# State products on four quarters of the array, logit sums one chunk later, column maxima joined on POOL

## The chip, the cores and the metric

The program runs on one core of a Trainium2 chip. The time is the device time of one execution in microseconds (us). Three runs of the kernel before took 564.08, 565.28 and 568.5 us; the median is 565.28 us.

## The reference

q, k and v have the shape 4 x 8 x 768 x 64 (batch, heads, sequence, head dimension), all float32. Three stages follow one another:

```
state = gamma[h] * state + k_t (outer) v_t ;  y_t = q_t . state / 8       # attention, per batch and head
x = y as 3072 tokens x 512
logits = x @ phi (512 x 32);  d = softmax over the 3072 tokens;  slot_input = d.T @ x
slot_out[e] = relu(slot_input[e] @ w1[e]) @ w2[e]                        # 8 experts, 4 slots each
x = softmax over the 32 slots of logits @ slot_out
out = sum over the top 2 of 8 experts (noisy gate) of weight * relu(x @ w1b[e]) @ w2b[e]
```

The first softmax runs over the tokens, so it needs a maximum for each of the 32 columns of the logits over all tokens.

## The kernel before, in words

**Chunks.** The sequence of each batch is cut into 6 chunks of 128 tokens, so there are 24 chunks, numbered t = 0 to 23. Chunk by chunk, attention is computed as products within the chunk and a product with the state that the earlier chunks left. The program is written out by hand for each engine; semaphores order the engines.

**TensorE, one chunk (`sequence_products`, L735).** In iteration t it issues, in this order: `scores` (L643) of chunk t+1, q.k for 8 heads with 64 contraction rows; `logit_parts_of` (L657) of chunk t-1, phi times x in four column tiles of 32; a wait for the state of this chunk (`state_ready`); `turn_x` (L675) of chunk t-1, four transposes of 128x128; `outputs`, which are the 8 state products (L684, not in the first chunk of a batch) and the 8 products of masked scores and v (L690), all into one bank of PSUM, `Y`; `logit_rows` (L664) of chunk t-1, which sums the four parts of the logits by one product with a stack of unit matrices; `update` (L697), the 8 products k.v for the state (not in the last chunk of a batch). Each float32 product shows as two records in the trace, so 8 products are x16.

**State products.** Head 2n uses the array's rows and columns 0 to 63, head 2n+1 rows and columns 64 to 127. Two of the four 64x64 quarters of the array are used.

**Other engines.** DVE masks the scores (L1182), scales y into `x_t` (`keep_x_t`, L1189) and keeps the state (`keep_state`, L1198 and L1201). ACT copies the logit parts (L1009), the turned x (L1015) and the logits (L1017). POOL scales v by its decay (L531). SP loads q, k and v, two transfers of 512 KB for a chunk (L408), and between them the first stage's w1 in halves of 1024 KB (L440), 14 halves for the 21 chunks from 3 on. A chunk's k and v are loaded when the scores of the chunk two before are done, its q and k-by-token when the update four before is done.

**Column maxima.** The chunks form five groups, which end before chunks 4, 8, 14, 20 and 24. For each group DVE finds the maximum over its chunks for each partition (`find_max`, L1222, and a copy to four places, L1224), TensorE turns it (`turn_max`, L704), DVE reduces it and joins it with the older maximum (`join_max`, L1230 to L1233), TensorE spreads it to all partitions (`spread_max`, L710), DVE subtracts (`shift_cols`, L1241), ACT takes the exponential (L1022, L1024), and TensorE sums the slots (L719) and denominators (L731). For the last group this chain has nothing of attention left beside it.

**After attention** the products with w1 (L808) and w2 (L830) of the slots follow, then the gate, the sort by expert and the second expert stage (L940, L957). The loads of w2 and of the later weights are issued when buffers come free, and thus at points that move with the end of attention.

Of the kernel before, what the change touches and what calls it, by code (L numbers as in the profile page):

```python
# [12 lines left out]
ABSMAX = bass.bass_isa.ReduceOp.absmax  # L13


def build_program(nc, chunks, phi, w1a, w2a, w_gate, w_noise, noise, w1b, w2b, consts, out, dims):
    B, H, S, D = dims
    NC = S // P
# [38 lines left out]
    with ExitStack() as ctx:  # L57
# [41 lines left out]
        logit_parts = work_tile(3, P)  # L99
# [38 lines left out]
        col_max = r_region[:, 3 * SZ:3 * SZ + P].rearrange("p (j s) -> p j s", j=REP)  # L138
# [49 lines left out]
        max_new = sb("max_new", [P, NG], F32)  # L188
        max_all = sb("max_all", [P, NG], F32)
# [3 lines left out]
        max_diag = sb("max_diag", [SL, SL], F32)  # L193
# [94 lines left out]
        col_max_turned = sem("col_max_turned")  # L288
        max_diag_ready = sem("max_diag_ready")
        max_spread = sem("max_spread")  # L290
# [76 lines left out]
        Y, ST, T_X, LG = range(4, 8)  # L367
# [158 lines left out]
        def _(pool):  # L526
# [29 lines left out]
            for c in range(2, NC):  # L556
                decay_chunk(0, c)
            with pool.Fori(1, B) as b:
                for c in range(NC):
                    decay_chunk(b, c)  # L560
# [7 lines left out]
            nc.gpsimd.memset(in_blocks, 0.0).then_inc(blocks_zeroed, 1)  # L568
            pool.wait_ge(slot_in_done, NG)
# [61 lines left out]
        def _(pe):  # L631
# [15 lines left out]
            def logit_parts_of(b, c):  # L647

                pe.wait_ge(x_t_ready, b * NC + c + 1)
                if not (isinstance(b, int) and b * NC + c == 0):  # L650
                    pe.wait_ge(logits_kept, b * NC + c)
                for g in group_ending(b * NC + c - 3):
                    if g < NG - 2:

                        pe.wait_ge(den_kept, g + 1)
                for d in range(DC):
                    last = nc.tensor.matmul(bank[LG][d * SL:(d + 1) * SL, 0:P], phi_sb[:, d, :], x_t[:, c % 2, d, :],  # L657
                                            start=True, stop=True)
                last.then_inc(parts_done, 1)

            def logit_rows(b, c):

                pe.wait_ge(parts_kept, b * NC + c + 1)
                nc.tensor.matmul(bank[LG][:, P:P + SL], logit_parts, stack, start=True, stop=True).then_inc(logits_done, 1)  # L664

            def turn_x(b, c):

                if not (isinstance(b, int) and b * NC + c == 0):
                    pe.wait_ge(x_kept, b * NC + c)
                for g in group_ending(b * NC + c - 3):  # L670
                    if g < NG - 2:

                        pe.wait_ge(slot_in_kept, g + 1)
                for d in range(DC):
                    last = nc.tensor.transpose(bank[T_X][:, d * P:(d + 1) * P], x_t[:, c % 2, d, :], ident[:, :])  # L675
                last.then_inc(x_turned, 1)

            def outputs(b, c):

                if c > 0:  # L680
                    for n in range(NP):
# [5 lines left out]
                pe.wait_ge(v_decayed, b * NC + c + 1)  # L687
                pe.wait_ge(probs_ready, b * NC + c + 1)
                for h in range(H):
                    last = nc.tensor.matmul(bank[Y][h % 2 * D:(h % 2 + 1) * D, h // 2 * P:(h // 2 + 1) * P],  # L690
                                            v_dec[c % 2][:, h * D:(h + 1) * D], probs[c % 2][:, h % 2, h // 2, :],
                                            start=(c == 0 and h < 2), stop=(h >= H - 2), skip_group_check=True)
                last.then_inc(y_ready, 1)

            def update(b, c):
                for h in range(H):
                    last = nc.tensor.matmul(bank[ST][h % 2 * D:(h % 2 + 1) * D, h // 2 * D:(h // 2 + 1) * D],  # L697
                                            k_in[(b * NC + c) % QK_DEPTH][:, h * D:(h + 1) * D], v_dec[c % 2][:, h * D:(h + 1) * D],
                                            start=(h < 2), stop=(h >= H - 2), skip_group_check=True)
                last.then_inc(update_done, 1)  # L700

            def turn_max(b):
                pe.wait_ge(col_max_ready, b + 1)
                nc.tensor.transpose(bank[ST][:, 2 * P:3 * P], col_max.rearrange("p j s -> p (j s)"),  # L704
                                    ident[:, :]).then_inc(col_max_turned, 1)

            def spread_max(b):
                pe.wait_ge(max_diag_ready, b + 1)
                pe.wait_ge(consts_ready, 4)
                nc.tensor.matmul(bank[ST][:, 3 * P:3 * P + SL], ones[0:SL, :], max_diag[:, :], start=True,  # L710
                                 stop=True).then_inc(max_spread, 1)
# [12 lines left out]
            def den_sums(g, kept):  # L724
                pe.wait_ge(logits_kept, kept)
# [4 lines left out]
                for c in range(end - first):  # L730
                    last = nc.tensor.matmul(bank[LG][c % REP * SL:(c % REP + 1) * SL, 480:482], exp_of(g)[:, c, :],  # L731
# [3 lines left out]
            def sequence_products(b):  # L735
                for c in range(NC):
                    before_b, before_c = (b, c - 1) if c > 0 else (b - 1, NC - 1)
                    if (b, c) == (0, 0):
# [9 lines left out]
                    if (b, c) == (0, 1):  # L748
                        pe.wait_ge(phi_full, 16)
                        pe.wait_ge(ident_full, 16)  # L750
                    if c > 0 or b > 0:
# [5 lines left out]
                    t = b * NC + c  # L757
# [5 lines left out]
                    if c > 0 or b > 0:  # L763
                        logit_rows(before_b, before_c)
                    if c < NC - 1:
                        for g in group_ending(t - 1) + (group_ending(t - 2) if c == 0 else []):

                            pe.wait_ge(max_diag_ready, g + 1)
                        for g in group_ending(t - 2) + (group_ending(t - 3) if c == 0 else []):

                            pe.wait_ge(cols_shifted, g + 1)
                        update(b, c)
                    for g in group_ending(t - 3):
                        if g < NG - 2:
                            slot_sums(g, range(GROUPS[g][1] - GROUPS[g][0]), bank[T_X], t)
                            den_sums(g, t)
# [4 lines left out]
            logit_parts_of(B - 1, NC - 1)  # L781
            turn_x(B - 1, NC - 1)
            logit_rows(B - 1, NC - 1)


            slot_sums(NG - 2, range(REP), bank[0], GROUPS[NG - 2][1])
# [896 lines left out]
```

## Time and profile before

| | |
|---|---|
| median of 3 runs | 565.28 us |
| the profiled execution: its span | 563.3 us |
| PE busy | 515.7 us (92%) |
| DVE, ACT, POOL busy | 277.4, 187.4, 257.3 us |
| chunks (12 to 130 us): PE busy, DMA share | 116.75 of 118 us, 0.91 |
| second expert stage, L957 busy | 296.1 us |

The profile is of one execution, and for it the span is the time that is given. PE is the matrix engine's products, PEld its weight loads, which overlap them. "Issue" as a cause of idle time means that the engine waited for nothing that the profile shows. A number behind `x` counts records. The DMA share is the mean busy share of 16 DMA engines.

### The profile page before, as it was taken

To read this page: it belongs to the slowest core of one execution; us is meant where nothing else is said; L and a number is where in the kernel's file an instruction comes from. 1 tells how busy PE (TensorE), PEld (TensorE's weight loads), DVE (VectorE), ACT (ScalarE), POOL (GpSimd) and SP (SyncE) were. 2 spreads that over 40 slices of the span, in tenths; PEclk is the share of its full clock that TensorE was granted. 3 is DMA by queue.
4 is the path that set the end of the run, shared out by engine and by line. 5 is a ranking of instruction groups with operands and counts; after the bars stand their busy time and mean duration, and the time that the engine had idled before them with its cause. 6 is when DMAs were issued, how large, how long until landed. Compare 5 with 4: busy or idle time off the path is not lost.

```text
span 563.3 us, 13506 instructions
## 1 busy us (share of the span) xinstructions
PE 515.7 (92%) x4845; PEld 305.0 (54%) x4846; DVE 277.4 (49%) x449; ACT 187.4 (33%) x345; POOL 257.3 (46%) x216
## 2 busy tenths in 40 slices
PE   4999999998895767789999999999999999999992
PEld 4787878775465534345545454545454545454541
DVE  1665756573710388863363637373737242424240
ACT  0122222222000354763636464545452222222220
POOL 1212221220100003735587778777778757566632
PEclk9999999999799578979999999999999999999998
DMA  7899999877899999915435552222232342424310
GB/s 261 308 324 392 313 353 340 334 287 266 347 430 424 427 400 412 311 50 200 156 94 177 191 189 44 41 40 54 42 54 43 49 56 42 57 38 54 45 18 2
DMA packets 32358, 107.91 MB, mean 192 GB/s; under 512 B 11567, under 2 KB 12831, under 8 KB 27840
## 3 DMA queue, kind: packets, MB, share of 16 engines
q1 hardware_dynamic: 18144, 92.89, 43.5%
q0 software_dynamic: 14176, 14.49, 14.3%
q8 instruction: 26, 0.43, 0.3%
q14 instruction: 12, 0.10, 0.1%
HBM read 93.87 MB, written 29.43 MB: 219 GB/s over the span
## 4 chain that ended last, share of the span: by engine, by line
PE 82%; DVE 7%; DMA 4%; issue 3%; ACT 1%; POOL 1%; SPq 0%; DVEq 0%; POOLq 0%
PE ps L957 49%; PE ps L940 4%; PE ps L690 4%; PE ps L643 4%; PE ps L684 3%; PE ps L808 3%; PE ps L830 3%; PE ps L675 3%; PE ps L697 2%; DMA w_region<-chunks 2%; DMA w_region<-moe_w 2%; PE ps L664 1%; PE ps L657 1%; PE ps L719 1%; ACT r_region L1067 1%
## 5 line engine op out<-in xcount | busy, mean ns | idle before, releaser
L957 PE MATMUL ps<-w_region,s_region 128*128 (+1 forms) x1320 | 296.1, 381 | 1.1 <-ACT s_region L1136 1.1
L957 PEld LDWEIGHTS ps<-w_region,s_region 128*128 128x128 f16 x1320 | 127.4, 98 | 145.7 <-issue 4.2
L1559 DVE SCALAR_TENSOR_TENSOR s_region<-ps,s_region 128x1024 f16<-128x1024 f32 x55 | 67.3, 1224 | 148.4 <-ACT s_region L1136 148.3
L1136 ACT ACTIVATE s_region<-ps 128x1024 f16<-128x1024 f32 x55 | 56.3, 1023 | 183.2 <-PE ps L940 178.8
L594 POOL DMA_INDIRECT out<-s_region,rec_region x41 | 56.1, 1367 | 53.2 <-DVE s_region L1588 50.0
L600 POOL DMA_INDIRECT out<-s_region,rec_region x42 | 67.8, 1614 | 16.4 <-issue 12.0
L588 POOL DMA_INDIRECT rec_region<-records,idx x55 | 60.0, 1090 | 24.9 <-issue 16.3
L531 POOL TENSOR_TENSOR s_region<-w_region,s_region 128x512 f32<-128x512 f32 x22 | 22.9, 1042 | 90.5 <-PE ps L697 71.7
L940 PEld LDWEIGHTS ps<-s_region,sw_region 128*128 (+1 forms) x440 | 29.4, 98 | 15.3 <-issue 2.7
L1588 DVE TENSOR_SCALAR s_region<-ps,rec_region,y_scale 128x512 f32<-128x512 f32 x42 | 33.8, 804 | 6.9 <-PE ps L957 5.4
L940 PE MATMUL ps<-s_region,sw_region 128*128 128x128 f16 x440 | 34.1, 221 | 2.0 <-ACT sw_region L1089 2.0
L1189 DVE TENSOR_TENSOR sw_region<-ps,s_region 128x512 f32<-128x512 f32 x24 | 16.6, 692 | 35.0 <-PE ps L690 35.0
L1360 DVE SCALAR_TENSOR_TENSOR w_region<-w_region,w2b_scale 128x2048 f16<-128x2048 f32 x14 | 32.6, 2342 | 0.0
L564 POOL PARTITION_ALL_REDUCE w2b_sum<-w2b_sum x8 | 3.2, 402 | 56.6 <-ACT w_region L1067 55.9
L1049 ACT ACTIVATE w_region<-w_region,w2b_scale 128x2048 f16<-128x2048 f32 x14 | 27.8, 2001 | 0.7 <-DVE w2b_scale L1354 0.7
L594 POOL DMA_INDIRECT out<-r_region,rec_region x13 | 19.5, 1504 | 16.4 <-DVE r_region L1588 15.6
L1009 ACT ACTIVATE s_region<-ps 128x128 f32<-128x128 f32 x24 | 6.7, 277 | 52.8 <-PE ps L657 52.8
L1067 ACT ACTIVATE r_region<-w_region 128x2048 f16<-128x2048 f32 x12 | 22.9, 1912 | 0.5 <-DMA w_region<-moe_w 0.4
L600 POOL DMA_INDIRECT out<-r_region,rec_region x13 | 20.7, 1592 | 4.8 <-issue 3.7
L643 PE MATMUL ps<-w_region 64*128 64x128 f32 x192 | 15.8, 310 | 5.1 <-DMA w_region<-chunks 5.0
L1182 DVE TENSOR_TENSOR sw_region<-ps,s_region 128x512 f32<-128x512 f32 x24 | 15.4, 680 | 9.2 <-PE ps L643 9.2
L1182 DVE TENSOR_TENSOR s_region<-ps,s_region 128x512 f32<-128x512 f32 x24 | 15.4, 681 | 6.5 <-PE ps L643 6.5
(241 smaller groups left out, 576.4 us busy)
## 6 DMA issues: line engine op xcount, KB each, us to landing
w_region<-moe_w SPq DMA_DIRECT2D x11, 2048.0 KB, 10.0
w_region<-chunks SPq DMA_DIRECT2D x34, 512.0 KB, 6.5
w_region<-moe_w SPq DMA_DIRECT2D x16, 1024.0 KB, 9.2
w_region<-moe_w SPq DMA_DIRECT2D x24, 512.0 KB, 17.1
s_region<-moe_w SPq DMA_DIRECT2D x4, 2048.0 KB, 16.8
sw_region<-chunks SPq DMA_DIRECT2D x12, 512.0 KB, 6.2
s_region<-moe_w SPq DMA_DIRECT2D x2, 1024.0 KB, 8.0
s_region<-moe_w SPq DMA_DIRECT2D x1, 1536.0 KB, 6.5
```

What stands on the lines that cost most here:

```text
L588: nc.gpsimd.indirect_dma_start(rec_i[:, i * RW:(i + 1) * RW], None, records[:, :], bass.IndirectOffsetOnAxis(ap=idx[:, i:i + 1], axis=0), ...
L594: nc.gpsimd.indirect_dma_start(out[:, :], bass.IndirectOffsetOnAxis(ap=rec_i[:, i * RW + SL + 1:i * RW + SL + 2], axis=0), y_sb[i % DEPTH] ...
L600: nc.gpsimd.indirect_dma_start(out[:, :], bass.IndirectOffsetOnAxis(ap=rec_i[:, i * RW + SL + 2:i * RW + SL + 3], axis=0), y_sb[i % DEPTH] ...
L643: last = nc.tensor.matmul(bank[SC[c % 2][i]][:, n * P:(n + 1) * P], kt_in[g % KV_DEPTH][rows, n, :], qt_in[g % QK_DEPTH][rows, n, :], star ...
L940: last = nc.tensor.matmul(bank[2 + 2 * r + f // 4][:, f % 4 * P:(f % 4 + 1) * P], sw_parts[:, bass.ds(e, 1), f * P:(f + 1) * P].rearrange( ...
L957: last = nc.tensor.matmul(bank[6 + r], h[:, r, f, :], w2b_parts[:, bass.ds(o, 1), part, f, :].rearrange("p e m -> p (e m)"), start=(first ...
L1067: nc.scalar.activation(unused, w2b_in[e][:, part * UNIT // W2B_SUMS:(part + 1) * UNIT // W2B_SUMS], ACT.Abs, accum_out=w2b_sum[:, 0, e, pa ...
L1136: nc.scalar.activation(h_hi[:, r, :, :].rearrange("p c t -> p (c t)").rearrange("p (a n) -> p a n", a=2), ps[:, 2 + 2 * r:4 + 2 * r, :], A ...
L1182: last = nc.vector.tensor_tensor(probs[c % 2][:, i, :, :], bank[SC[c % 2][i]][:, :].rearrange("p (n t) -> p n t", n=NP), causal[:, :].unsq ...
L1360: last = nc.vector.scalar_tensor_tensor(out=w2b_parts[:, e, 1, chunks, :], in0=w2b_in[e].rearrange("p (c m) -> p c m", c=FC)[:, chunks, :] ...
L1559: nc.vector.scalar_tensor_tensor(out=h_lo[:, r, :, :].rearrange("p c t -> p (c t)").rearrange("p (a n) -> p a n", a=2), in0=ps[:, 2 + 2 * ...
L1588: nc.vector.tensor_scalar(y_sb[r], bank[6 + u % 2], rec[:, bass.ds(i * RW + SL, 1)], y_scale[:, bass.ds(o, 1)], ALU.mult, ALU.mult).then_i ...
```

## The change

- The 8 state products take all four quarters: the row half is still the head's parity i, the column half is now `half` = n % 2. The output of parity i goes to a bank of its own, `Y + i`, so y takes half of each of two banks. `keep_x_t` reads both in one instruction. The order of the heads in x changes by that; phi, w1 and the decay table are permuted to match on the host.
- `logit_rows` of chunk t-2 now stands behind `turn_x` of chunk t-1, ahead of the outputs, and not of chunk t-1 behind the outputs. The logit parts lie in bank `Y + 1` and have two copies in SBUF; the summed logits lie in the bank of the state.
- The wait for the state stands behind `turn_x`, not ahead of it.
- New waits on TensorE: `outputs` for `parts_kept`, `update` for `logits_kept`, and ahead of the w1 stage for the last `den_kept`. ACT copies the logits of chunk t-1 behind the turned x of chunk t.
- `turn_max`, `spread_max` and `join_max` are gone. POOL joins the column maxima over the partitions by one `partition_all_reduce` of 128x32 for each group; DVE joins it with the older maximum and works out the gap between the two by three small instructions.

```diff
-                        for i in range(2):
-                            part = slice(i * D, (i + 1) * D)
-                            nc.tensor.matmul(bank[Y][part, n * P:(n + 1) * P], state[part, n, :],
-                                             qt_in[(b * NC + c) % QK_DEPTH][part, n, :],
-                                             start=(n == 0), stop=False, skip_group_check=True)
+                pe.wait_ge(parts_kept, t)
+                    for m in range(2):
+                        for half in range(2):
+                            for i in range(2):
+                                rows, n = slice(i * D, (i + 1) * D), 2 * m + half
+                                nc.tensor.matmul(y_of[i][half * D:(half + 1) * D, m * P:(m + 1) * P], state[rows, n, :],
+                                                 qt_in[t % QK_DEPTH][rows, n, :],
+                                                 start=(m == 0), stop=False, skip_group_check=True)
...
+            def update(b, c):
+                t = b * NC + c
+                if t > 1:
+                    pe.wait_ge(logits_kept, t - 1)
...
-                        logit_parts_of(before_b, before_c)
-                        if c > 0:
-                            pe.wait_ge(state_ready, b * (NC - 1) + c)
-                        turn_x(before_b, before_c)
-                    for g in group_ending(t - 1):
-                        turn_max(g)
-                    for g in group_ending(t - 2):
-                        spread_max(g)
+                    logit_parts_of(t - 1)
+                    turn_x(t - 1)
+                    if c > 0:
+                        pe.wait_ge(state_ready, b * (NC - 1) + c)
+                    if t > 1:
+                        logit_rows(t - 2)
                     outputs(b, c)
-                        logit_rows(before_b, before_c)
                     if c < NC - 1:
                         update(b, c)
...
+            def join_col_max(g):
+                pool.wait_ge(col_max_ready, g + 1)
+                nc.gpsimd.partition_all_reduce(col_max[:, 1 if g > 0 else 2, :], col_max[:, 0, :], P, MAX).then_inc(col_max_joined, 1)
+            for t in range(2, NT):
+                decay_chunk(t // NC, t % NC)
+                for g in group_ending(t - 2):
+                    join_col_max(g)
...
+            def shift_cols(g):
+                dve.wait_ge(col_max_joined, g + 1)
                 if g > 0:
+                    link(nc.vector.tensor_tensor(max_at(g), col_max[:, 1, :], max_at(g - 1), ALU.max))
...
+                if g > 0:
+                    link(nc.vector.tensor_tensor(gap_stack, max_at(g - 1), max_at(g), ALU.subtract))
+                    link(nc.vector.tensor_tensor(gap_stack, gap_stack, stack, ALU.mult))
+                    nc.vector.tensor_reduce(gap[:, g:g + 1], gap_stack, AX_X, ALU.add).then_inc(gap_found, 1)
...
+            def keep_logits(t):
+                act.wait_ge(logits_done, t + 1)
+                nc.scalar.activation(logits[:, t, :], rows_at, ACT.Copy).then_inc(logits_kept, 1)
             def keep_chunk(t):
...
                 act.wait_ge(x_turned, t + 1)
                 nc.scalar.activation(x_home(t), bank[T_X][:, :], ACT.Copy).then_inc(x_kept, 1)
+                if 0 < t < NT - 1:
+                    keep_logits(t - 1)
```

## Rows read from the trace of the kernel before

**Rows 1.** The page: the span, and the granted clock in 40 slices.
```profile
span 563.3 us, 13506 instructions
...
PEclk9999999999799578979999999999999999999998
```

**Rows 2.** The page: shares of the chain that ended last, by line.
```profile
PE ps L957 49%; PE ps L940 4%; PE ps L690 4%; PE ps L643 4%; PE ps L684 3%; PE ps L808 3%; PE ps L830 3%; PE ps L675 3%; PE ps L697 2%; DMA w_region<-chunks 2%; DMA w_region<-moe_w 2%; PE ps L664 1%; PE ps L657 1%; PE ps L719 1%; ACT r_region L1067 1%
```

**Rows 3.** Windows: busy us by engine; last three granted clock, DMA share, GB/s.
```profile
12.00:130.00 118.00, 116.75 (x1712) 92.17 (x1712) 73.05 (x131) 25.53 (x76) 22.92 (x22) 1.00 0.91 331
142.00:147.00 5.00, 3.96 (x35) 1.55 (x34) 3.67 (x9) 0.84 (x1) 0.29 (x1) 0.50 0.88 354
155.00:200.00 45.00, 31.26 (x669) 24.25 (x661) 9.71 (x31) 8.39 (x12) 0.37 (x1) 0.84 1.00 423
```

**Rows 4.** Waits, 12 to 130 us: total us, times, longest.
```profile
PEld ps L675 <- DVE s_region L1201: 4.6, 15, 0.4
...
PEld ps L643 <- DMA w_region<-chunks: 1.0, 2, 0.7
```

**Rows 5.** Timeline of one iteration, 82.4 to 87.7 us: start, us, instruction.
```profile
82.50 0.97 PEld L643 LDWEIGHTS ps<-sw_region,w_region 64*128 64x128 f32 x16
...
83.07 0.91 DVE L1201 TENSOR_TENSOR s_region<-s_region 128x256 f32<-128x256 f32 x1
83.59 0.16 PEld L657 LDWEIGHTS ps<-sw_region,s_region 128*32 128x32 f32 x8
...
84.03 0.42 PEld L675 LDWEIGHTS ps<-ident_stack,sw_region 128*128 128x128 f32 x4 [0.29 <-DVE s_region L1201]
...
84.08 0.28 ACT L1009 ACTIVATE s_region<-ps 128x128 f32<-128x128 f32 x1 [1.90 <-PE ps L657]
...
84.62 0.85 PEld L684 LDWEIGHTS ps<-sw_region,s_region 64*64 64x64 f32 x16 [0.17 <-issue]
...
84.79 0.60 ACT L1015 ACTIVATE w_region<-ps 128x512 f32<-128x512 f32 x1 [0.43 <-PE ps L675]
85.64 0.85 PEld L690 LDWEIGHTS ps<-sw_region,s_region 128*64 128x64 f32 x16 [0.17 <-issue]
...
86.67 0.30 PEld L664 LDWEIGHTS ps<-ident_stack,s_region 128*128 128x128 f32 x2 [0.17 <-issue]
...
86.79 0.69 DVE L1189 TENSOR_TENSOR sw_region<-ps,s_region 128x512 f32<-128x512 f32 x1 [1.60 <-PE ps L690]
87.00 0.55 PEld L697 LDWEIGHTS ps<-s_region,sw_region 128*64 128x64 f32 x16
...
87.11 0.20 ACT L1017 ACTIVATE r_region<-ps 128x32 f32<-128x32 f32 x1 [1.73 <-PE ps L664]
```

**Rows 6.** Timeline of PEld, behind the last turn: L664 lies between these.
```profile
134.52 0.42 PEld L675 LDWEIGHTS ps<-ident_stack,sw_region 128*128 128x128 f32 x4 [0.20 <-issue]
...
135.32 0.16 PEld L719 LDWEIGHTS ps<-w_region,r_region 128*32 128x32 f32 x8
```

**Rows 7.** Timeline of a chunk in which a maximum is spread.
```profile
64.58 0.29 PEld L710 LDWEIGHTS ps<-max_diag,ones 32*128 32x128 f32 x2 [0.17 <-issue]
```

**Rows 8.** Windows where the DMA engines are full, and issues of w1.
```profile
27.00:32.00 5.00, 4.92 (x80) 3.90 (x78) 3.10 (x6) 1.07 (x3) 0.85 (x2) 1.00 1.02 414
42.00:47.00 5.00, 4.86 (x76) 3.98 (x74) 2.71 (x6) 1.27 (x4) 1.80 (x2) 1.00 1.01 409
...
w_region<-moe_w SPq DMA_DIRECT2D x14, 1024.0 KB, 9.1
```

**Rows 9.** Timeline of DVE, last group: maximum found, and shift.
```profile
135.93 0.38 DVE L1222 TENSOR_REDUCE r_region<-r_region 128x32 f32<-128x128 f32 x1 [1.82 <-ACT r_region L1017]
...
138.44 0.29 DVE L1241 TENSOR_TENSOR r_region<-r_region,ps 128x128 f32<-128x128 f32 x1 [0.67 <-PE ps L710]
```

**Rows 10.** Lines L564 (2 columns) and L578 (4 columns): ns min/median/max.
```profile
L564 POOL PARTITION_ALL_REDUCE w2b_sum<-w2b_sum x8: 312/323/872, 198.2 to 408.3; - x8
...
L578 POOL PARTITION_ALL_REDUCE sw_sum<-sw_sum x2: 338/750/1163, 211.8 to 231.5; - x2
```

More of the change, by code:

```diff
@@ L366, in build_program @@
         SC = ((0, 1), (2, 3))
-        Y, ST, T_X, LG = range(4, 8)
+        Y, T_X, ST = 4, 6, 7
+        y_of = [bank[Y + i][:, 0:2 * P] for i in range(2)]
+        y_all = ps[:, Y:Y + 2, 0:2 * P]
+        parts_at = bank[Y + 1][:, 2 * P:3 * P]
+        den_at = bank[Y + 1][:, 400:402]
+        state_at = bank[ST][:, 0:NP * D]
+        rows_at = bank[ST][:, NP * D:NP * D + SL]
         def wait_consumed(engine, b, c):
@@ L645, in scores, with logit_parts_of @@
                 last.then_inc(scores_ready, 1)
[L647 to L652, printed above, removed]
+            def logit_parts_of(t):
+                pe.wait_ge(x_t_ready, t + 1)
+                if t > 0:
+                    pe.wait_ge(parts_kept, t)
+                for g in group_ending(t - 3):
                     if g < NG - 2:
@@ L656, in logit_parts_of, with logit_rows, turn_x @@
                 for d in range(DC):
-                    last = nc.tensor.matmul(bank[LG][d * SL:(d + 1) * SL, 0:P], phi_sb[:, d, :], x_t[:, c % 2, d, :],
+                    last = nc.tensor.matmul(parts_at[d * SL:(d + 1) * SL, :], phi_sb[:, d, :], x_t[:, t % 2, d, :],
                                             start=True, stop=True)
                 last.then_inc(parts_done, 1)
[L661 to L670, printed above, removed]
+            def logit_rows(t):
+                pe.wait_ge(parts_kept, t + 1)
+                if t > 0:
+                    pe.wait_ge(logits_kept, t)
+                nc.tensor.matmul(rows_at, logit_parts[t % 2], stack, start=True, stop=True).then_inc(logits_done, 1)
+            def turn_x(t):
+                if t > 0:
+                    pe.wait_ge(x_kept, t)
+                for g in group_ending(t - 3):
                     if g < NG - 2:
@@ new lines, in outputs @@
+                pe.wait_ge(v_decayed, t + 1)
+                pe.wait_ge(probs_ready, t + 1)
+                for m in range(2):
+                    for i in range(2):
+                        for half in range(2):
+                            n = 2 * m + half
+                            h = 2 * n + i
+                            last = nc.tensor.matmul(y_of[i][half * D:(half + 1) * D, m * P:(m + 1) * P],
+                                                    v_dec[c % 2][:, h * D:(h + 1) * D], probs[c % 2][:, i, n, :],
+                                                    start=(c == 0 and m == 0), stop=(m == 1), skip_group_check=True)
@@ L722, in slot_sums, with den_sums @@
                     last.then_inc(slot_in_done, 1)
[L724 to L725 removed]
+            def den_sums(g, read):
+                pe.wait_ge(x_t_ready, read)
                 if g == NG - 1:
@@ L780, in _ @@
                 sequence_products(b)
[L781 to L786, printed above, removed]
-            turn_max(NG - 1)
-            slot_sums(NG - 2, range(REP, GROUPS[NG - 2][1] - GROUPS[NG - 2][0]), bank[0], GROUPS[NG - 2][1])
+            logit_parts_of(NT - 1)
+            logit_rows(NT - 2)
+            turn_x(NT - 1)
+            logit_rows(NT - 1)
+            slot_sums(NG - 2, range(GROUPS[NG - 2][1] - GROUPS[NG - 2][0]), bank[0], GROUPS[NG - 2][1])
             den_sums(NG - 2, NT)
-            spread_max(NG - 1)
             slot_sums(NG - 1, range(REP), bank[1], NT)
@@ L1272, in sequence_copies @@
                     for g in group_ending(t - 1):
-                        join_max(g)
+                        find_max(g)
                     for g in group_ending(t - 2):
@@ L1276, in sequence_copies @@
                     keep_x_t(b, c)
-                    for g in group_ending(t):
-                        find_max(g)
                     if c < NC - 1:
@@ L1672 @@
     arrays["moe2_noise"] = noise_by_token(arrays["moe2_noise"])
+    for name in ("moe_phi", "moe_w1"):
+        arrays[name] = by_quarter(arrays[name], inputs["q"].shape[1])
     for name in ("moe_w1", "moe_w2", "moe2_w1", "moe2_w2"):
```

129 lines of the change are left out of this document (50 added, 79 removed).

## The prediction

> **What bounds the kernel now.** I read the chain of waits first [rows 2]: half of it is the second expert stage (L957), which the change does not touch; L643, L684, L690, L675, L697, L664 and L657 belong to the chunks. The windows [rows 3] then say what kind of stage the chunks are: from 12 to 130 us PE is busy 116.75 of 118 us at full clock, while the DMA engines are busy 0.91 of the time at 331 GB/s. So TensorE sets the pace, and the loads are close behind it. The waits [rows 4] agree: TensorE waits 4.6 us in all for the state (15 times) and 1.0 us for chunks. The timeline of one iteration [rows 5] gives the pace: from one L643 at 82.50 to the next (the 0.55 of L697 at 87.00, and a little) it is 5.12 us. Between 155 and 200 us the DMA engines are full at 423 GB/s [rows 3]; but those loads are released by points that follow the end of attention, so an earlier end moves them along, and I carry the saving to the end one for one.
>
> **State products.** In L684 16 weight loads take 0.85 us [rows 5], 53 ns each; L690, whose two column halves work at once, has the same rate, so L684 now runs two at a time, in 8 rounds of 0.109 us. L657 with four column tiles gets its 8 loads out in 0.16 us [rows 5], and its slot up to L675 is 0.44 us, of which 0.29 is waiting: four tiles do go at once there. With four quarters the state products need 4 rounds instead of 8: 0.44 us less for each of the 20 chunks that have them. **8.7 us.** Bounds: 0, if the quarters do not overlap four wide, and 8.7. I take 8.7, since the issue of L657 is fast enough and L643 already writes two banks from two row halves at the pace of two at once (0.97 us for 16).
>
> **Logit sums moved.** Now L664 sits between L690 and L697: weight loads of L690 end at 86.49, L697 begins at 87.00, 0.51 us. L690 and L697 have the same tile shape, 128*64, so without L664 about 0.07 us is left: 0.44 saved. Behind the turn, which has L664's own shape 128*128, it costs what the end of attention shows [rows 6]: from L675 to the next shape 0.80 us with L664 between, against 0.59 from L675 to L684 [rows 5], so 0.21. Net 0.23 us, 22 times: **5.1 us**. The 0.21 is a bound from above, because there L664 waited for ACT.
>
> **Waits.** The state's wait goes behind the turn. L675 waited 0.29 us [rows 5], but without any wait 0.20 stays [rows 6], so 0.09 for the 15 waits [rows 4]: **1.4 us**. What is late next: the state. After the last load of L690 (call it T) DVE does L1189 (ends T+0.9), L1198 and L1201 (0.91 us), ready at about T+2.35. TensorE does update 0.62, scores 1.09, parts 0.36, turn 0.49, so it asks at T+2.56. Cover 0.2 us; in group chunks the extra DVE work may eat it, some tenths in all. `outputs` waits for L1009, which ends 0.77 us after L657 starts [rows 5]; the products start at least 1.1 us after it: cover 0.3. `update` waits for the logits behind the 0.60 us copy of x: about 2.0 us after L657's start, asked at about 2.6: cover 0.6. Behind each of these waits everything on TensorE queues, so a cover that is gone costs its full length in each chunk. The DVE read of y over two banks is the same 512 elements: nothing.
>
> **Group work.** Four `spread_max` in the chunks cost 0.33 us each (64.58 to the L684 of 64.91) [rows 7], four `turn_max` about 0.1 each, a quarter of the turn's 0.42 [rows 5]: **1.7 us**. DVE loses about as many small instructions as it gains. POOL has idle time in every chunk. Sum on TensorE within the chunks: 8.7+5.1+1.4+1.7 = **16.9 us**.
>
> **What the loads allow.** A chunk is 1.05 MB, and 14 halves of w1 over 21 chunks [rows 8] add 0.70: 1.75 MB. The 22 iterations from 21.4 to 133.4 us average 5.09 us; less 16.9 they would be 4.32 us, which asks for 405 GB/s. Where the DMA engines are full they moved 409 to 414 [rows 8]; but the mean, 331 at a share of 0.91, is 364 at a share of one [rows 3]. So an iteration can be no shorter than 4.28 us by the best windows and 4.81 by the mean. The loads of a chunk are released two iterations ahead, by TensorE's own progress, so they cannot run ahead to even this out. I take the middle, 4.55 us: 22 x (5.09-4.55) = **12 us** saved, with bounds of 6.2 (mean rate) and 16.9 (never late). L643 will wait for the chunks, not 1 us in all but about 5.
>
> **End of attention.** From the end of the last L1222 (136.31) to the shift at 138.44 it is 2.13 us [rows 9]: copy, turn, three DVE steps, spread. After it is POOL's reduction, one join and two hand-overs. The reduction took 323 ns with 2 columns and 338 in the shorter of two with 4 [rows 10]. About 8 ns a column more gives 0.55 us for 32; in proportion to the columns 5.2 us. I take 0.55, because two and four columns hardly differ; then 0.8 in place of 2.13. The extra logit sum ahead of the last turn takes 0.2 of this back: **1.2 us** saved, with a bound of 3.3 lost.
>
> The Trainium skill (GPSIMD Engine Reference, Cross-partition — where GPSIMD wins) gives 247,699 ns for a reduction along the partitions of 128x2048, another instruction; an estimate from that page is 3.9 us for 32 columns, and with it the end of attention would lose about 2 us instead. The rows at 2 and 4 columns speak against such a price for this instruction, and no run here shows it at 32.
>
> **Sum.** 12.0 + 1.2 = 13.2 us off 563.3, so 550.1 for such an execution; the median of the runs lies 2.0 above the profiled span [rows 1], which gives **552 us**.
>
> **Rivals.** (A) The loads keep up: 16.9 + 1.2 + the cover of L664 = about 18 us, 547 us. For it: windows at 409 and 414. Against: the 0.91 mean. Chance 0.2. (B) The loads go at their mean rate: 6.2 + 1.2 = 7.4, 558 us. For it: it is what the loads did over 118 us, full windows included. Against: a share at few transfers in flight overstates the need. Chance 0.17. (C) The change does not do what it says: quarters of the same rows, with different moving data, go one after another. Then 8.2 + 1.2 = 9.4, and the loads do not bind: 556 us. L657 shows four column tiles at once, but nothing shows two by two. Chance 0.06. (D) Slower: POOL's reduction of 32 columns is slow. Its place is between `find_max` and `shift_cols`, which stands ahead of `keep_x_t` on DVE, for which TensorE waits in the next scores' shadow. About 4 us are free there; each further us costs one in each of four groups and one at the end. It eats the 13.2 us at 4 x (L-4) + (L-0.55) = 13.2, so L = 6.0 us, and at 8 us the kernel takes 563.3-13.2+23.5+2 = 576 us. For it: the one sample of 1163 ns; against: the other rows. Chance 0.04. The forecast has 0.50; the rest (0.03) is small losses of the covers, near no change. One more thing moves the time either way: a half-clock stretch like that at 142 to 147 us [rows 1, 3]; one of some 7 us more or less under TensorE-bound work is worth up to 3.4 us.
>
> **Range and chances.** From 545 (A with a kinder clock) to 560 (B with a stretch of half clock more), which leaves D and part of the rest out. About 1% (5.7 us) is what a measurement of this kernel can tell from no change. Faster by more: forecast, A, nearly all of C, two thirds of B: 0.86. Within 1%: 0.09. Slower: 0.05, D and a little.
>
> **What would show it.** L684: 16 loads in some 0.4 us, followed by L690 after 0.17. Update directly behind L690, with under 0.1 between. The L664 records behind the turn, about 0.2 us. An iteration at 4.3 to 4.4 where no chunk is late, and waits of L643 for chunks of about 5 us in total; DMA share near 1.0 up to the last chunk. The reduction under 1 us. It would be wrong if L684 keeps 0.85 (C), if L643 never waits or waits over 9 us (A, B), if DVE waits for POOL ahead of L1189 (D), or if L664 or the outputs wait for DVE or ACT in every chunk.

## The result, and the profile after

The median after is 598.38 us (595.14 to 601.88), against 564.68 us for the kernel before on the same chip (four runs; the 565.28 us ahead of the prediction is of the first three). The ratio is 1.060, with an interval of [1.053, 1.066]: the change makes the kernel 33.7 us slower. The forecast was 552 us.

The page of the profiled execution after (one digit of the clock row for each 15 us; the chain's shares by engine, then by line):

```profile
span 597.5 us, 13496 instructions
...
PEclk9996969989659977887999999999999999999998
...
PE 70%; DMA 14%; issue 10%; POOL 2%; DVE 1%; SPq 1%; ACT 0%; POOLq 0%; DVEq 0%
PE ps L958 47%; DMA w_region<-moe_w 7%; DMA w_region<-chunks 7%; PE ps L941 4%; PE ps L652 3%; PE ps L710 3%; PE ps L809 3%; PE ps L831 2%; PE ps L686 1%; SPq L505 1%; PE ps L732 1%; PE ps L700 1%; PE ps L721 1%; PE ps L867 1%; PE ps L666 1%
```

A tenth of the chain is now "issue", time in which an engine waits for nothing that the profile shows. The clock row has a 6, a 6 and an 8 inside the chunks (from 45, 75 and 120 us on), where [rows 1] has nines, and a 6 and a 5 from 149 to 179 us, at their end. The windows of the chunks (busy us of PE, PEld, DVE, ACT, POOL; granted clock, DMA share, GB/s), up to where the last chunk's products begin:

```profile
12.00:155.50 143.50, 109.79 (x1732) 88.29 (x1729) 68.02 (x129) 24.52 (x78) 25.00 (x27) 0.89 0.71 268
```

In [rows 3] PE was busy 0.99 of the stage; now it is 0.77, and the loads have fallen from 331 to 268 GB/s as well. So neither TensorE nor the loads set the pace, the two bounds that the forecast went by. What TensorE waited for in this stretch (total us, times, longest):

```profile
PE ps L710 <- POOL s_region L536: 18.0, 4, 5.0
PE ps L652 <- DMA w_region<-chunks: 8.6, 9, 1.8
PE ps L666 <- DVE sw_region L1201: 5.4, 4, 2.8
```

L710 are the products of masked scores and v (L690 of before), and L536 is POOL's scaling of v, which nobody waited for before. L652 are the scores, and L666 the products of phi and x, which need DVE's `keep_x_t` (L1201). "4 times" is the count of groups that end inside the chunks. So I looked at the two lines of POOL. First the reduction (L563), then the scaling (L536), each with the marks of a change of POOL's code, which its sequencer issues (POOLq, two records for each change); ns min/median/max, first and last start, and what ended the engine's idle time before it:

```profile
L563 POOLq MODIFY_POOL_CONFIG  x10: 9/11/17, 37.9 to 161.7; - x10
L563 POOL PARTITION_ALL_REDUCE r_region<-r_region x5: 450/452/452, 47.0 to 169.2; - x5
...
  issue: 31.5, 4
...
L536 POOLq MODIFY_POOL_CONFIG  x8: 99/99/99, 47.4 to 147.6; - x8
...
  issue: 27.9, 4
```

The reduction takes 0.45 us. But five times POOL's code is changed ahead of it, and four times changed back ahead of the next scaling. The timeline of the first group, with the last reduction:

```profile
36.66 1.04 POOL L536 TENSOR_TENSOR s_region<-w_region,s_region 128x512 f32<-128x512 f32 x1 [4.45 <-DMA w_region<-chunks]
46.99 0.45 POOL L563 PARTITION_ALL_REDUCE r_region<-r_region  x1 [9.29 <-issue]
54.53 2.04 POOL L536 TENSOR_TENSOR s_region<-w_region,s_region 128x512 f32<-128x512 f32 x2 [7.09 <-issue]
...
48.42 0.16 PEld L666 LDWEIGHTS ps<-sw_region,s_region 128*32 128x32 f32 x8 [2.98 <-DVE sw_region L1201]
...
49.51 0.73 PEld L700 LDWEIGHTS ps<-sw_region,s_region 64*64 64x64 f32 x16
55.62 1.57 PEld L710 LDWEIGHTS ps<-s_region 128*64 128x64 f32 x16 [5.38 <-POOL s_region L536]
...
55.64 0.33 SPq L413 DMA_DIRECT2D w_region<-chunks  x1
...
169.22 0.45 POOL L563 PARTITION_ALL_REDUCE r_region<-r_region  x1 [7.79 <-issue]
```

From the mark at 37.9 to the reduction at 46.99 pass 9.1 us; from the mark at 47.4 to the scaling at 54.53 pass 7.1 us. Three things hang on it. DVE waits for the reduction with the scaling of y queued behind, and TensorE's L666 waits 2.98 us for that. TensorE's L710 waits 5.38 us for the scaled v. And the next k and v are loaded only at 55.64: the loads wait for the scores, as told ahead of the prediction, and in both kernels for the scaling of v as well (`v_decayed`), since it reads the same buffer. TensorE comes out of each of the four waits for v at the lower of its two levels (1.2 GHz). Here the granted clock is 0.50 from 49.5 to 58 us and 1.00 again from 60 on, and L710 takes 1.57 us here, 0.85 at 2.4 GHz.

The change of code does not wait for the maxima. In the fourth group the last scaling ends at 140.95 us, the maxima are ready at 143.03 and the reduction starts at 147.17. DVE thus sees less of the forward change than POOL does: from the maxima to the end of the reduction it is 7.6, 6.7, 5.8 and 4.6 us in the four groups inside the chunks, and 8.2 in the last. The scaling of v has both changes ahead of it, and more than half of TensorE's idle time in this stretch, 18.0 of 33.7 us, is for it.

The Trainium skill (GPSIMD Engine Reference, Instruction dispatch) says that the first call to a freshly loaded kernel costs about 6 us, measured from this same mark less the wait for an event, with no instruction in the profile for it. The trace agrees in kind and mostly has more: POOL stands idle 6.2 to 9.3 us ahead of a reduction and 6.8 to 7.1 ahead of the scaling.

The same view of line L564 of the kernel before, whose first row stands in [rows 10], had one more:

```profile
L564 POOLq MODIFY_POOL_CONFIG  x2: 11/14/16, 142.5 to 142.5; - x2
```

There the mark is at 142.5 us and the first reduction runs at 198.2, with POOL waiting for ACT between them. That change of code was covered: nobody waited for it.

The rest of the change did what was forecast. One iteration after, undisturbed by loads or POOL (start, us):

```profile
102.72 0.97 PEld L652 LDWEIGHTS ps<-w_region 64*128 64x128 f32 x16
...
103.43 0.84 DVE L1213 TENSOR_TENSOR s_region<-s_region 128x256 f32<-128x256 f32 x1
103.82 0.16 PEld L666 LDWEIGHTS ps<-sw_region,s_region 128*32 128x32 f32 x8
104.17 0.42 PEld L686 LDWEIGHTS ps<-ident_stack,sw_region 128*128 128x128 f32 x4 [0.20 <-issue]
...
104.56 0.30 PEld L675 LDWEIGHTS ps<-ident_stack,s_region 128*128 128x128 f32 x2
104.90 0.43 PEld L700 LDWEIGHTS ps<-sw_region,s_region 64*64 64x64 f32 x16
105.50 0.85 PEld L710 LDWEIGHTS ps<-s_region 128*64 128x64 f32 x16 [0.17 <-issue]
106.32 0.60 PEld L721 LDWEIGHTS ps<-s_region,sw_region 128*64 128x64 f32 x16
106.99 0.30 PEld L652 LDWEIGHTS ps<-w_region 64*128 64x128 f32 x4
```

The 16 weight loads of the state products (L700) take 0.43 us, not 0.85 [rows 5]; the logit sums (L675) stand behind the turn (L686); the update (L721) follows L710 directly; and the iteration takes 106.99 - 102.72 = 4.27 us, where it took 5.12.

### The profile page after: what moved, and what is told of

It reads as the page before. It is cut to its first block, busy times and chain, and to the rows that moved or that the text cites. A ratio compares the mean times of both kernels' runs of the same rounds, so it can differ in the third digit from the quotient of the medians.

```text
span 597.5 us, 13496 instructions
## 1 busy us (share of the span) xinstructions
PE 508.1 (85%) x4830; PEld 300.2 (50%) x4831; DVE 271.4 (45%) x446; ACT 185.1 (31%) x345; POOL 258.8 (43%) x221
## 4 chain that ended last, share of the span: by engine, by line
PE 70%; DMA 14%; issue 10%; POOL 2%; DVE 1%; SPq 1%; ACT 0%; POOLq 0%; DVEq 0%
PE ps L958 47%; DMA w_region<-moe_w 7%; DMA w_region<-chunks 7%; PE ps L941 4%; PE ps L652 3%; PE ps L710 3%; PE ps L809 3%; PE ps L831 2%; PE ps L686 1%; SPq L505 1%; PE ps L732 1%; PE ps L700 1%; PE ps L721 1%; PE ps L867 1%; PE ps L666 1%
## 5 line engine op out<-in xcount | busy, mean ns | idle before, releaser
L609 POOL DMA_INDIRECT out<-s_region,rec_region x42 | 67.8, 1614 | 16.0 <-issue 12.3
L536 POOL TENSOR_TENSOR s_region<-w_region,s_region 128x512 f32<-128x512 f32 x22 | 22.9, 1046 | 87.3 <-DMA w_region<-chunks 29.0
L1201 DVE TENSOR_TENSOR sw_region<-ps,s_region 128x512 f32<-128x512 f32 x24 | 16.5, 689 | 45.5 <-PE ps L710 45.5
L710 PE MATMUL ps<-s_region 128*64 128x128 f32 x192 | 16.6, 328 | 18.0 <-POOL s_region L536 18.0
L603 POOL DMA_INDIRECT out<-r_region,rec_region x13 | 19.3, 1482 | 16.6 <-DVE r_region L1592 15.9
L652 PE MATMUL ps<-w_region 64*128 64x128 f32 x192 | 16.7, 323 | 11.0 <-DMA w_region<-chunks 9.6
L710 PEld LDWEIGHTS ps<-s_region 128*64 128x64 f32 x192 | 13.1, 165 | 20.5 <-POOL s_region L536 19.1
L867 PE MATMUL ps<-w_region,slot_out_t 128*32 128x256 f32 x192 | 14.5, 452 | 10.4 <-DMA w_region<-moe_w 10.4
```

Source lines behind the costliest of these rows:

```text
L603: nc.gpsimd.indirect_dma_start(out[:, :], bass.IndirectOffsetOnAxis(ap=rec_i[:, i * RW + SL + 1:i * RW + SL + 2], axis=0), y_sb[i % DEPTH] ...
L609: nc.gpsimd.indirect_dma_start(out[:, :], bass.IndirectOffsetOnAxis(ap=rec_i[:, i * RW + SL + 2:i * RW + SL + 3], axis=0), y_sb[i % DEPTH] ...
L652: last = nc.tensor.matmul(bank[SC[c % 2][i]][:, n * P:(n + 1) * P], kt_in[g % KV_DEPTH][rows, n, :], qt_in[g % QK_DEPTH][rows, n, :], star ...
L710: last = nc.tensor.matmul(y_of[i][half * D:(half + 1) * D, m * P:(m + 1) * P], v_dec[c % 2][:, h * D:(h + 1) * D], probs[c % 2][:, i, n, : ...
```

## The experiments

Three theories at first; the expectations call them S, W and R. **Code** (S): the loss is the change of POOL's code, five times forth and four times back. **Collision** (W): it is something else of the change (the new waits of `outputs` and `update`, late loads), and POOL only shows it. **Reduction** (R): the reduction itself is slow; its 0.45 us in the trace speak against that. The later experiments ask what the rest of the change is worth and where it goes.

**The reduction out.** POOL copies the column instead; the join over the partitions is left out.

```diff
-  nc.gpsimd.partition_all_reduce(col_max[:, 1 if g > 0 else 2, :], col_max[:, 0, :], P, MAX)...
+  nc.gpsimd.tensor_copy(col_max[:, 1 if g > 0 else 2, :], col_max[:, 0, :])...
```

> The changed kernel, with POOL's reduction over the partitions (L563) replaced by a plain copy of the same 128x32 on POOL. It leaves the join of the maxima over the partitions out; everything else is as in the changed kernel. Theory S (change of code): POOL changes its code between the scaling of v (L536) and the reduction and back, some 7 to 9 us each way, and TensorE waits for the late scaling and the late loads. Then this kernel has no such pauses and takes 548 to 555 us. Theory W (the new waits for ACT and the shared banks cost the time): it stays above 585 us. Theory R (the reduction itself takes the time): also 548 to 555 us, so this run does not tell R from S.

Measured: 551.24 us, ratio to before 0.978 [0.971, 0.984]. One instruction, 0.45 us long and used five times, is worth 598.38 - 551.24 = 47.1 us, 9.4 us for each. No mark of a code change is left on that line. The kernel before took 564.68 us beside the one and 564.06 beside the other, so 0.6 us of the 47 may be the chip. The same stretch of the chunks in this kernel, and TensorE's waits in it:

```profile
12.00:119.76 107.76, 99.17 (x1721) 81.86 (x1721) 70.06 (x129) 24.43 (x78) 24.72 (x26) 1.00 0.97 368
```
```profile
PE ps L652 <- DMA w_region<-chunks: 7.2, 10, 1.6
PE ps L666 <- DVE sw_region L1201: 1.2, 2, 0.9
```

This splits the loss. The last chunk's products begin at 119.76 here and at about 155.5 after, 35.7 us apart. PE's idle time in the stretch is 107.76 - 99.17 = 8.6 us here and 143.50 - 109.79 = 33.7 after: 25.1 us are waits, of which the rows name 18.0 for the scaling of v, 4.2 more for DVE and 1.4 more for loads. PE's busy time is 109.79 against 99.17 for the same work: the other 10.6 us go with the lower clock (0.89 against 1.00). The last group adds what is left: from L710's last start to the first product with w1 it is 9.1 us here (119.76 to 128.89) and 20.1 after (155.49 to 175.58), 11.0 us. 35.7 + 11.0 = 46.7, of 47.1.

**The scaling of v on DVE.** The whole change stays, the reduction too; POOL has nothing else to do in the chunks, so its code need not change back.

```diff
-            for t in range(2, NT):
-                decay_chunk(t // NC, t % NC)
-                for g in group_ending(t - 2):
-                    join_col_max(g)
+            for g in range(NG - 1):
+                join_col_max(g)
...
+            def decay_late(t):
+                ...
+                nc.vector.tensor_tensor(v_dec[t % 2]..., v_in[r]..., v_dec_by..., ALU.mult).then_inc(v_decayed, 1)
...
+                    if t + 2 < NT:
+                        decay_late(t + 2)
```

> The whole change, with the scaling of v from chunk 2 on moved from POOL to DVE (one instruction of about 0.68 us behind keep_state), so that POOL runs nothing in the chunks but the reductions. Theory S: one change of code ahead of the first reduction, none after; each reduction 0.45 us, 549 to 556 us, with DVE L1201-like steps at 0.42 and no longer 0.9 us since POOL no longer works beside them. Theory R: the pauses stay where the reductions are, above 580 us. Theory W: above 585 us.

Measured: 552.05 us, 0.971 [0.962, 0.980], single runs from 545.8 to 554.2. The reductions are there and do their work, 0.43 us each, and the loss is gone. POOL changes its code once, at 12.3 us, long before the first reduction. Even the clearing of a buffer between the last two reductions forces no change:

```profile
122.87 0.98 POOL L574 MEMSET sw_region<- 128x1056 f32 x1 [9.96 <-PE ps L684]
124.03 0.43 POOL L563 PARTITION_ALL_REDUCE r_region<-r_region  x1 [0.19 <-DVE r_region L1237]
```

So it is the scaling, a TENSOR_TENSOR, that needs the other code, and not whatever stands beside a reduction. Theory R falls as well.

**The old kernel with four unread reductions.** Their input is zeroed, and nobody reads what they give; the scaling of v is queued behind them.

```diff
+            def unread_join(g):
+                nc.gpsimd.partition_all_reduce(unread[:, 1 + g % 2, :], unread[:, 0, :], P, MAX)...
...
+            for t in range(2, NT):
+                decay_chunk(t // NC, t % NC)
+                for g in group_ending(t - 2):
+                    unread_join(g)
```

> The kernel before, with four reductions of 128x32 added on POOL at the places that the change gives them in the chunks; they work on zeros and nothing waits for their results. Theory S: 14 to 17 us of pause on POOL at each of the four, TensorE then waits for the scaling of v 3 to 6 us at each, and the loads start later: 575 to 590 us. Theories R and W: 4 times 0.45 us on an engine with idle time, 563 to 567 us.

Measured: 595.6 us, 1.056 [1.049, 1.063], more than the 575 to 590 that I expected. Nothing of the change is in this kernel but the alternation on POOL (and its loop written out), and it loses 31.5 us. POOL's timeline, then its waits in the chunks:

```profile
46.19 0.45 POOL L562 PARTITION_ALL_REDUCE r_region<-r_region  x1 [9.26 <-issue]
53.53 2.04 POOL L535 TENSOR_TENSOR s_region<-w_region,s_region 128x512 f32<-128x512 f32 x2 [6.89 <-issue]
```
```profile
POOL r_region L562 <- issue: 30.3, 4, 9.3
POOL s_region L535 <- issue: 28.4, 4, 7.4
```

The same changes, 6.1 to 9.3 us forth and 6.9 to 7.4 back. TensorE waits 16.8 us for the scaled v here, though nobody reads the reductions. Collision falls: new waits, quarters and moved sums are not needed for the loss.

**Code changes with nobody behind them.** The kernel with the scaling on DVE, and behind each of the first four reductions one unread product of 128x32 on POOL, which forces the change back.

```diff
             for g in range(NG - 1):
                 join_col_max(g)
+                nc.gpsimd.tensor_tensor(unread, unread, unread, ALU.mult).then_inc(unread_done, 1)
```

> As the kernel with the scaling of v on DVE, but POOL multiplies 128x32 unused zeros (a TENSOR_TENSOR) behind each of the first four reductions, and nothing waits for that product. POOL changes its code twice for each group again, but the groups are 17 us or more apart and nobody stands behind it. Theory S: the change costs only where somebody waits behind it, so 550 to 556 us, with pauses of 7 to 9 us in POOL's timeline. Rival: the changes cost by themselves (through the DMA engines or the clock): 4 x 7 us or more, above 575 us. If the change back is late for the next reduction, a few us more than 552.

Measured: 560.44 us, 0.991 [0.987, 0.994], 8.4 us above the kernel without these products and more than the 550 to 556 that I expected. POOL's timeline, and one row of TensorE:

```profile
52.61 0.23 POOL L574 TENSOR_TENSOR r_region<-r_region 128x32 f32<-128x32 f32 x1 [11.37 <-issue]
62.03 0.45 POOL L566 PARTITION_ALL_REDUCE r_region<-r_region  x1 [9.19 <-issue]
...
121.83 0.23 POOL L574 TENSOR_TENSOR r_region<-r_region 128x32 f32<-128x32 f32 x1 [8.10 <-issue]
...
132.03 0.45 POOL L566 PARTITION_ALL_REDUCE r_region<-r_region  x1 [7.20 <-issue]
...
133.42 0.14 PEld L738 LDWEIGHTS ps<-w_region,r_region 128*32 128x32 f32 x3 [7.49 <-ACT r_region L1037]
```

Four changes back lie inside the chunks, 8.1 to 11.4 us long, and so do four forth, of which three end before their maxima are ready. They cost nothing that shows: from the first reduction to the last chunk's products it is 79.9 us (40.78 to 120.66), against 80.2 (39.45 to 119.68) in the kernel without them and 79.5 in a second profile of that kernel. Only the fifth change forth, with nothing left beside it, is paid: 7.49 us of TensorE, and the w1 stage starts at 138.39 instead of 129.05. The expectation had left it out. So it is not the change of code that costs, but what waits behind it.

**Two groups of five.** The change with the reduction for groups 1 and 2 alone, a copy for the others (the join over partitions is left out there).

```diff
+                if g in (1, 2):
+                    nc.gpsimd.partition_all_reduce(col_max[:, 1, :], col_max[:, 0, :], P, MAX)...
+                else:
+                    nc.gpsimd.tensor_copy(...)
```

> The changed kernel, with the reduction kept for the second and the third group and a plain copy on POOL in place of it for the first, fourth and fifth (which leaves the join over partitions out there). Theory S says that the loss of 47 us between this kernel with five copies (551) and with five reductions (598) is additive, 9.4 us for each: 570 us, 565 to 575. If one place made the loss (the end of attention, or the first use) it would be near 551 or near 598.

Measured: 572.09 us, 1.014 [1.010, 1.017]; two groups cost 20.9 us, 10.4 each, near the 9.4 of all five. So the price goes by the group, and no single place makes the loss.

**Two quarters.** The kernel with the scaling on DVE, its state products back on two quarters of the array (the columns again by the head's parity, the order of the heads as before).

```diff
-  nc.tensor.matmul(y_of[i][half * D:(half + 1) * D, m * P:(m + 1) * P], state[rows, n, :],
+  nc.tensor.matmul(y_of[m][rows, half * P:(half + 1) * P], state[rows, n, :],
```

> As the kernel with the scaling of v on DVE, but with the state products on two quarters of the array again (head parity sets row half and column half), and the order of the heads as before. If TensorE sets the pace of the chunks, 20 x 0.43 = 8 to 9 us more than that kernel; if the loads do, 2 to 5 us more.

Measured: 555.42 us, 0.983 [0.977, 0.989], 3.4 us above the kernel with four quarters. The two intervals overlap, so both were run again, side by side.

> The kernel with the whole change and the scaling of v on DVE once more, in more rounds and on one chip with its two-quarter variant: 550 to 554 us.

> The two-quarter variant of it, in more rounds: if the loads take back more than half of the 8.7 us of the four quarters, 553 to 557 us; if TensorE set the pace, 559 to 562.

Measured: four quarters 550.47 us, 0.975 [0.973, 0.977]; two quarters 556.74 us, 0.985 [0.983, 0.987]. The quarters are worth 6.3 us here, 3.4 in the first pair. On TensorE alone they save 0.43 us in each of 20 chunks, 8.6 us; this row is from the first kernel with two:

```profile
108.49 0.85 PEld L698 LDWEIGHTS ps<-w_region,s_region 64*64 64x64 f32 x16
```

The rest goes to the loads, 2.3 us here: less than the half that the last expectation asked for, though its time came out in the range. The windows of the second kernel with four quarters, what its scores waited for, and the same in the second with two:

```profile
12.00:116.00 104.00, 96.99 (x1690) 80.24 (x1690) 77.36 (x149) 23.58 (x75) 1.76 (x4) 1.00 0.98 371
```
```profile
PEld ps L650 <- DMA w_region<-chunks: 7.9, 12, 1.2
```
```profile
PEld ps L650 <- DMA w_region<-chunks: 5.5, 7, 1.9
```

The faster TensorE waits 2.4 us more for chunks, at a DMA share of 0.98. In the first pair it was 9.2 against 4.6 us, 4.6 more. So the waits account for about both gains, 8.6 - 2.4 = 6.2 and 8.6 - 4.6 = 4.0; why they differ so from pair to pair is not shown.

**Five of 14 halves of w1 later.** If the loads bind, fewer bytes beside the chunks should let attention end sooner. Five halves go behind the last chunk, the gate's matrices later still.

```diff
+            LATE = 5
-                more = (g - 2) * 2 * (E - 1) // (NT - 3)
+                more = (g - 2) * (2 * (E - 1) - LATE) // (NT - 3)
...
+            for half in range(ahead, 2 * (E - 1)):
+                w1a_half(half // 2, half % 2, w1a_early)
```

> The kernel with the scaling of v on DVE; 5 of the 14 halves of w1 are loaded behind the last chunk instead of between chunks, and the two gate matrices (32-byte rows) behind attention. If the loads set the pace of the chunks (7 us of waits of L650 for chunks in that kernel), attention ends 3 to 6 us earlier and, if the later halves are there in time, the kernel takes 546 to 550 us against 552. If TensorE set it, or if the late halves are waited for, 551 to 556.

Measured: 556.52 us, 0.985 [0.982, 0.988], 4.5 us slower than with all 14 beside the chunks (552.05, and 550.47 the second time). Attention hardly ends sooner, not by the 3 to 6 us that I expected: the w1 stage starts at 126.99, against 129.05 and 127.29 in the two profiles with all 14. And w2 then comes late:

```profile
PEld ps L831 <- DMA w_region<-moe_w: 10.2, 5, 3.2
```

The DMA engines stay at a share of 1.01 between 155 and 200 us in both kernels (420 and 415 GB/s). The bytes were only moved, to a place where they cost more.

**All 14 later**, a single run, to see TensorE's own pace in the chunks.

```diff
-            LATE = 5
+            LATE = 2 * (E - 1)
```

> As the kernel with 5 halves of w1 behind the last chunk, but with all 14 there: the chunks' own loads are all that the DMA engines do. It shows TensorE's own pace: if the steps of the forecast are right (16.9 us less on TensorE), the last products of L710 start at 115 to 117 us, with hardly a wait of the scores for chunks. The kernel as a whole is 10 us or more slower than 552 us, since the w1 products then wait for 14 MB.

Measured: 571.59 us (no interval). The last chunk's products start at 113.24 us, sooner than the 115 to 117 that I expected, with two waits for chunks, 1.4 us in all, against 117.9 to 119.8 in the three kernels with all 14 halves beside the chunks and 132.28 before. That is 132.28 - 113.24 = 19.0 us sooner, of which the loads keep 4.6 to 6.5 in the others. The scaling of v on DVE is in the 19.0 too, and the next run shows that it moves this point by itself.

**Control: the old kernel with the scaling on DVE.**

```diff
-            for c in range(2, NC):
-                decay_chunk(0, c)
-            with pool.Fori(1, B) as b: ...
+                    if t + 2 < NT:
+                        decay_late(t + 2)
```

> Control: the kernel before, with nothing changed but the scaling of v from chunk 2 on moved to DVE. TensorE sets the pace of its chunks and waits 4.6 us for the state, which L1201 at 0.42 instead of 0.9 would give back in part: 560 to 566 us. A gain of 10 us or more here would mean that the 552 of the other kernel comes from this move and not from the change.

Measured: 563.58 us, 0.998 [0.996, 1.001]. By itself that move does not show in the time, so what the kernel with the scaling on DVE gains is the change's. It did bring TensorE to the last chunk's products at 129.13 instead of 132.28, likely since DVE makes the state sooner (see the last section). Of these 3.2 us no more than 2.4 reached the end by the interval, and I did not follow the rest.

**The best version** is the whole change with the scaling of v on DVE: 550.47 us, 2.5% faster than before.

## Why the prediction was wrong

**The step that failed** is "POOL has idle time in every chunk", in the group work, with the price in the end of attention, "I take 0.55". The idle time was there (nothing on any engine waited for POOL's scaling of v before), and 0.45 us was measured for the reduction, inside the 0.55. What was priced was the instruction, not what stands between it and its neighbours. In the new place it alternates with the scaling of v, and each alternation changes POOL's code: 6 to 9 us forth, about 7 back. The step that should have followed was the one the text makes for every other engine, to ask what is queued behind the new wait: it named DVE's wait, and not that the next scaling of v sits behind the reduction on POOL, with TensorE and the loads of k and v behind that.

**Rival D** had the right place for half of it, between `find_max` and `shift_cols`. It asked for a slow instruction, though, and its formula gives only the forward half. With the longest, L = 9.3 + 0.45 = 9.75 us, it yields 4 x 5.75 + 9.2 = 32 us. With what DVE saw, 7.6, 6.7, 5.8, 4.6 and 8.2 us, it yields 9 in the chunks and 8 at the end. Measured are 35.7 and 11.0: the larger part in the chunks is the wait for v behind the change back, and the lower clock after it, of which D says nothing. Its chance of 0.04 rested on the durations of [rows 10] alone. The row with the two marks in the old kernel could have raised it; there the change stood far ahead of its use, which is why it looked free.

**State products**: right. 0.43 us for 16 loads, as 4 rounds in place of 8. Rival C is out.

**Logit sums moved and waits**: right in kind, and larger than forecast. From L690 to the update it was 1.36 us [rows 5] and is 0.82 now, and from the turn to the state products it was 0.59 and is 0.73: 0.40 us saved for each chunk, not 0.23. The iteration is 4.27 us where the loads do not bind (5.12 - 0.44 - 0.23 - 0.09 = 4.36 forecast). None of the new waits shows in the kernels without the change of code, beyond 1.2 us in all for `x_t` (reduction out).

**Sum on TensorE**: 16.9 us forecast. PE's busy time up to the last chunk's products is 99.17 us with the reduction out, where POOL still scales v, and was 118.40 before: 19.2 us less. The kernel with all of w1 late came 19.0 us sooner. The logit sums alone saved 22 x 0.17 = 3.7 us more than forecast, so the other terms together saved some 1.5 us less. The same stretch of the kernel before:

```profile
12.00:132.28 120.28, 118.40 (x1733) 93.44 (x1733) 73.63 (x132) 26.41 (x78) 22.92 (x22) 1.00 0.91 329
```

**What the loads allow**: right in size. Forecast was 12 us off the chunks; measured, by the start of the last chunk's products, 12.5 (reduction out), 12.6 and 14.4 (scaling on DVE, twice). The DMA share is 0.97 to 0.98 at 364 to 371 GB/s. TensorE's weight loads waited 7.9 to 9.2 us for chunks where I had said about 5, so the pace between late chunks was faster than thought and the waits longer; 9.1 and 9.2 are even past the "over 9 us" that was to speak for B. The 4.55 us of an iteration was the middle between two bounds and was not worked out, so that 12 came so close is partly luck. Rivals A (547) and B (558) stay on either side of 550.5.

**End of attention**: 10.98 us before; 9.1 with a copy, 9.4 with the reduction in place. That saves 1.6 to 1.9, against 1.2. From the maxima to the shift it is 0.79 us with the reduction in place, against 0.8 forecast. (The bound of 3.3 us lost leaves out the 0.2 of the extra logit sum; it should be 3.5.)

**One for one**: right to 1 or 2 us, for the loss as well. The first product with w1 came 32.3 us later than before (175.58 against 143.26), the whole kernel 33.7; with the reduction out 14.4 sooner (128.89) and 13.4. It does not hold for the control, which came there 3.3 us sooner (139.91) and gained 2.4 at most.

With the code change out of the way the prediction's sum holds: 552 forecast, 551.2, 552.1 and 550.5 measured. In part that is two misses that offset each other, TensorE's saving too small and its waits for chunks too small. One overlooked cost on POOL was 3.5 times the whole gain (47.1 against 564.68 - 551.24 = 13.4 us).

## What to carry to other kernels

On POOL a `partition_all_reduce` among elementwise products cost its duration and a change of code on either side. Look for MODIFY_POOL_CONFIG beside such instructions in the trace, and ask how long before its use it stands and who is queued behind it. If the change can't be covered, keep POOL to one kind of work in that stage and give the other to an engine with time to spare: here DVE took the scaling of v and 46 to 48 us came back. Here the DMA engines were full on both sides of the end of attention, and moving bytes from one side to the other gained nothing.

## What the runs showed that was not expected

**The code changes**: 6.1 to 9.3 us of idle time ahead of a reduction. Back to a TENSOR_TENSOR it was 6.8 to 7.4 us where the loads stood still because of it (DMA share 0.00 to 0.24), and 8.1 to 11.4 in the kernel with the unread products, where they went on (0.94 to 0.99). Full DMA engines may stretch the change, but the share alone does not decide it: of the changes forth one took 6.2 us at a share of 0.91 and one 9.3 at 0.88. No run tried this by itself. POOL's copy between two products needs no change, and the clearing of a buffer needs none behind a product nor, as shown above, between two reductions.

**DVE beside POOL**: the same instruction, two inputs of 128x256 f32 in SBUF, takes about twice as long where it runs beside POOL's scaling of v. Before it took 0.91 us [rows 5], after 0.84 (in the iteration above). With POOL out of the chunks:

```profile
54.88 0.42 DVE L1211 TENSOR_TENSOR s_region<-s_region 128x256 f32<-128x256 f32 x1
```

In the profile after, DVE took 0.42 us for it as well, at 58.95 us, where POOL was idle. So moving POOL's work to DVE cost DVE less than the 0.68 us of the moved instruction: 0.42 to 0.49 us of it came back in this one.
